# The opening of an attention block: constants built inside it, two heads prepared in separate PSUM banks, similarities ahead of scores, a weight load behind the head loop

## The reference, cut to what matters

```python
# B, H, S, D = 2, 8, 768, 64; 16 clusters
q_assign = argmax(einsum('bhsd,hcd->bhsc', q / |q|, c / |c|), axis=-1)   # k_assign likewise
mask = q_assign[:, :, :, None] == k_assign[:, :, None, :]
scores = where(mask, D ** -0.5 * q @ k.T, -1e9)
attn = softmax(scores) @ v
x = moe_1(attn, expert_emb, tau, w1, w2)      # top-1 of 8 experts
out = moe_2(x, w_gate, w1, w2)                # all 8 experts
```

## Time and profile before

| | us |
|---|---|
| median of three runs | 1681.98 |
| lowest and highest | 1680.38, 1683.75 |
| the profiled execution, its own time | 1681.38 |
| its span | 1679.4 |
| PE busy in the span | 1594.5 (95%) |
| DVE, ACT, POOL busy | 1196.2, 771.0, 277.6 |

### The profile page before, as it was taken

One profiled execution on the slowest core, in us unless ns is written; L12 is line 12 of the kernel. 1 busy time (PEld: TensorE's weight loads), 2 busy tenths in 40 slices (PEclk: granted clock), 3 DMA queues, 4 the chain that ended last, 5 costly groups with the idle time before them and its releaser, 6 DMA issues.

```text
span 1679.4 us, 27324 instructions
## 1 busy us (share of the span) xinstructions
PE 1594.5 (95%) x8554; PEld 1417.0 (84%) x8554; DVE 1196.2 (71%) x1996; ACT 771.0 (46%) x1361; POOL 277.6 (17%) x283
## 2 busy tenths in 40 slices
PE   3999999957999998999999999999999999999998
PEld 3899988846777777898998998998998998998997
DVE  3799999976899997487665665666666666666664
ACT  2576677775888885223333332322323323323331
POOL 1111111114443335010010010010010010010002
PEclk9999999988999999999999999999999999999999
DMA  3322222133353341011010010010010010010001
GB/s 71 103 58 56 56 56 57 37 86 113 138 201 123 119 150 39 13 43 33 26 51 26 25 50 26 25 50 26 25 50 26 25 50 26 25 50 25 25 0 75
DMA packets 123697, 94.90 MB, mean 57 GB/s; under 512 B 66344, under 2 KB 101160, under 8 KB 123632
## 3 DMA queue, kind: packets, MB, share of 16 engines
q1 hardware_dynamic: 121152, 86.06, 17.1%
q0 software_dynamic: 2480, 8.13, 1.6%
HBM read 87.88 MB, written 6.29 MB: 56 GB/s over the span
## 4 chain that ended last, share of the span: by engine, by line
PE 73%; DVE 2%; ACT 1%; POOL 1%; issue 1%; DMA 1%; DVEq 0%; ACTq 0%; POOLq 0%
PE moe_bank L1170 11%; PE moe_bank L1168 11%; PE moe_bank L1169 11%; PE moe_bank L1145 9%; PE moe_bank L1148 9%; PE moe_bank L1147 9%; PE moe_bank L1089 2%; PE moe_bank L1091 2%; PE moe_bank L1090 2%; PE moe_bank L1102 2%; PE moe_bank L1104 2%; PE moe_bank L1103 2%; PE moe_bank L1041 1%; ACT moe_h_rows L1315 1%; DMA moe_x_rows<-tokens,moe_token_of_item 1%
## 5 line engine op out<-in xcount | busy, mean ns | idle before, releaser
L1705 DVE SCALAR_TENSOR_TENSOR all_x<-moe_bank,all_x 128x512 f32<-128x512 f32 x336 | 251.5, 749 | 127.5 <-PE moe_bank L1170 124.7
L1145 PE MATMUL moe_bank<-moe_x_t_hi,all_w_hi 128*128 128x384 f32 x896 | 305.1, 340 | 3.0 <-DVE all_w_lo L727 2.9
L1148 PE MATMUL moe_bank<-moe_x_t_hi,all_w_lo 128*128 128x384 f32 x896 | 303.2, 338 | 0.0
L1147 PE MATMUL moe_bank<-moe_x_t_lo,all_w_hi 128*128 128x384 f32 x896 | 302.2, 337 | 0.0
L1168 PE MATMUL moe_bank<-moe_w_hi,moe_h_hi 128*128 128x512 f32 x768 | 301.1, 392 | 0.0
L1169 PE MATMUL moe_bank<-moe_w_lo,moe_h_hi 128*128 128x512 f32 x768 | 300.7, 392 | 0.0
L1170 PE MATMUL moe_bank<-moe_w_hi,moe_h_lo 128*128 128x512 f32 x672 | 265.0, 394 | 0.0
L1145 PEld LDWEIGHTS moe_bank<-moe_x_t_hi,all_w_hi 128*128 128x128 f32 x896 | 168.6, 188 | 14.0 <-issue 3.6
L1147 PEld LDWEIGHTS moe_bank<-moe_x_t_lo,all_w_hi 128*128 128x128 f32 x896 | 168.6, 188 | 11.3
L1148 PEld LDWEIGHTS moe_bank<-moe_x_t_hi,all_w_lo 128*128 128x128 f32 x896 | 168.4, 188 | 0.0
L1868 POOL TENSOR_TENSOR moe_w_sums<-moe_dense_w_raw 128x256 f32<-128x256 f32 x32 | 23.7, 740 | 853.2 <-DVE all_w_lo L727 853.2
(11 more groups left out here) (262 smaller groups left out, 3123.7 us busy)
## 6 DMA issues: line engine op xcount, KB each, us to landing
all_w_raw<-in_moe_w SPq DMA_DIRECT2D x8, 2048.0 KB, 7.6
moe_w_raw<-in_moe_w SPq DMA_DIRECT2D x8, 2048.0 KB, 9.2
moe_dense_w_raw<-in_moe_w SPq DMA_DIRECT2D x64, 256.0 KB, 3.0
moe_dense_w_raw<-in_moe_w SPq DMA_DIRECT2D x32, 512.0 KB, 3.5
attn_q_raw<-in_q SPq DMA_DIRECT2D x32, 192.0 KB, 3.4
attn_k_raw<-in_k SPq DMA_DIRECT2D x32, 192.0 KB, 3.9
attn_v_raw<-in_v SPq DMA_DIRECT2D x16, 192.0 KB, 3.8
tokens<-all_x SPq DMA_DIRECT2D x32, 96.0 KB, 2.0
```

Of the source, the lines that this page charges most:

```text
L1145: pe.matmul(out, hi[:, s, k, :], XH[chunk][:, x, k, :], start=(start and k == 0), stop=False, skip_group_check=True)
L1147: pe.matmul(out, hi[:, s, k, :], XL[chunk][:, x, k, :], start=False, stop=False, skip_group_check=True)
L1148: mm = pe.matmul(out, lo[:, s, k, :], XH[chunk][:, x, k, :], start=False, stop=(stop and k == 1), skip_group_check=True)
L1705: dve.scalar_tensor_tensor(acc, y, PROB[:, row, bass.ds(at, 1)], acc, ALU.mult, ALU.add).then_inc(y_added, 1)
```

## The change

The constants are built by POOL within the attention block, so the barrier between the two blocks is gone and each user waits for the `made` semaphore. SP issues the loads of head 0 first, with one semaphore each for q, k and v. The rows and tau go out on ACT's queue. ACT loads the table of the exponential early with a tiny activation (`TABLE`). PE runs `warm(8)` and `warm(4)`, 512-column matmuls on ones whose result nobody reads. The stages of heads 0 and 1 go to different banks of `ps_p`, `ps_t`, `ps_s` and `ps_o`, so that they don't wait for each other. The similarities of head 0 come ahead of the first scores. The first diagonal moves from POOL to DVE. SP issues the load of `W1R` behind its loop, and ACT waits for it at step 4 of the last part.

```diff
-    with nc.Block() as block:
-        @block.gpsimd
-        def _(pool):
...
-            pool.wait_ge(made, 9 + H - 1)
-    return c, scratch_at
+    return c, scratch_at, mem.sem("const_made")
+def build_constants(pool, c, made):
...
-            rows.load(sp)
-            load(0, 0)
+            for half in range(2):
+                sp.dma_start(QR[0][:, :, half, :], qd[0:1].rearrange("o p t d -> p (o t) d")).then_inc(first_q, 16)
+            for half in range(2):
+                sp.dma_start(KR[0][:, :, half, :], kd[0:1].rearrange("o p t d -> p (o t) d")).then_inc(first_k, 16)
+            sp.dma_start(VR[0][:], vd[0:1].rearrange("o p t d -> p (o t) d")).then_inc(first_v, 16)
             load(1, 1)
...
-            sp.dma_start(W1R[:, 0:DC, :], w1[0].rearrange("(c p) f -> p c f", p=P)).then_inc(w1_loaded, 16)
             with sp.Fori(2, G // 2) as i:
...
+            sp.dma_start(W1R[:, 0:DC, :], w1[0].rearrange("(c p) f -> p c f", p=P)).then_inc(w1_loaded, 16)
...
+            pe.wait_ge(made, 3)
+            warm(WARM[0])
+            pe.wait_ge(made, IDENT)
+            pe.wait_ge(first_q, 32)
+            transpose_raw(0, 0, 4).then_inc(prep_ready, 1)
+            transpose_raw(0, 4, 2, ps_t[:, 0], 4)
+            pe.wait_ge(first_k, 32)
+            transpose_raw(0, 6, 2, ps_t[:, 0], 4).then_inc(prep_ready, 1)
+            transpose_raw(0, 8, 4, ps_t[:, 1]).then_inc(prep_ready, 1)
+            pe.wait_ge(rows.step, rows.FIRST)
+            pe.transpose(ps_o[:, 0:P], unit[:].rearrange("p o d -> p (o d)"), c["ident"][:]).then_inc(cent_ready, 1)
+            warm(WARM[1])
+            pe.wait_ge(cent_split, 4)
+            pe.wait_ge(prep_lo, 3)
+            similarities(0, 0, ps_o[:, P:P + 2 * T * NC], 0)
+            similarities(0, 0, ps_o[:, P:P + 2 * T * NC], T).then_inc(prep_ready, 1)
+            pe.wait_ge(raw_loaded[1], LOADS)
+            transpose_raw(1, 0, 4, ps_s[1][:, 0]).then_inc(prep_ready, 1)
+            transpose_raw(1, 4, 4, ps_s[1][:, 1]).then_inc(prep_ready, 1)
+            transpose_raw(1, 8, 4, ps_t[:, 1]).then_inc(prep_ready, 1)
+            scores(0, 0, 0)
+            pe.wait_ge(diag_ready, 1)
+            key_ids(ps_t[:, 0], 0)
+            key_ids(ps_p[:], 3)
+            pe.wait_ge(prep_lo, 5)
+            scores(1, 1, 0)
+            pe.wait_ge(kid_ready, 2)
+            pe.wait_ge(prep_lo, 6)
+            similarities(1, 1, ps_p[:], 0)
             pe.wait_ge(rows.step, rows.DONE)
-            pe.transpose(ps_t[:, 0, 0:P], unit[:].rearrange("p o d -> p (o d)"), c["ident"][:]).then_inc(cent_ready, 1)
-            scores(0, 0, 0)
-            scores(1, 1, 0)
-            pe.wait_ge(cent_split, 4)
-            for stage in range(3, 7):
-                prep(0, 0, stage)
-            for stage in range(4):
-                prep(1, 1, stage)
-            pe.wait_ge(max_done, 1)
-            scores(2, 2, 0)
...
+            rows.load(act)
+            act.dma_start(TAU[:, 0:1], tau.rearrange("(o n) -> o n", o=1).broadcast_to([P, 1])).then_inc(tau_loaded, 16)
             rows.roots(act)
-            for stage in range(3):
-                prep(0, 0, stage)
+            act.wait_ge(made, 4)
+            act.activation(TABLE[:], c["rank16"][:, 0:1], ACT.Exp)
...
-            act.wait_ge(w1_loaded, 16)
             for s in range(2, 12):
                 step(G // 2 - 1, s)
+                if s == 4:
+                    act.wait_ge(w1_loaded, 16)
```

More of the change, by code:

```diff
@@ L146, in scale, with write @@
         dve.wait_ge(step, self.SUMS + 6)
[L147 to L150, removed]
+    def write(self, dve, j):
+        rows, outs = self.arrays[j]
+        for out in outs:
+            raw = self.raw[j][:].rearrange("r (h d) -> r h d", d=DH) if len(out.shape) == 3 else self.raw[j][:]
+            dve.tensor_scalar(out, raw, self.s[0:rows.shape[0], 2, j:j + 1], None, ALU.mult).then_inc(self.step, 1)
 def newton(dve, step, at, x, r, out, tmp):
@@ L165, in newton, with attention @@
     dve.reciprocal(out, tmp).then_inc(step, 1)
-def attention(nc, c, q, k, v, centroids, expert_emb, tau, w1, X, L, xs, W1R, W1H, w1_loaded, w1_hi, x_stored):
+def attention(nc, c, made, q, k, v, centroids, expert_emb, tau, w1, X, L, xs, W1R, W1H, w1_loaded, w1_hi, x_stored):
     with ExitStack() as stack:
@@ L309, in _, with transpose_raw, similarities, key_ids @@
         def _(pe):
-            def transpose_raw(g, j, first, n):
+            def transpose_raw(j, first, n, out=None, at=None):
+                out, at = out if out is not None else ps_p[:], first if at is None else at
                 for m in range(first, first + n):
                     src = (QR if m < T else KR)[j][:, m % T].rearrange("p o d -> p (o d)")
-                    mm = pe.transpose(ps_p[:, (m - first) * P:(m - first + 1) * P], src, c["ident"][:])
+                    mm = pe.transpose(out[:, (m - at) * P:(m - at + 1) * P], src, c["ident"][:])
+                return mm
+            def similarities(g, j, out, first):
+                cols = bass.ds((g % H) * NC, NC)
+                for m in range(first, first + T):
+                    sims = out[:, m * NC:(m + 1) * NC]
+                    if m < T:
+                        pe.matmul(sims, HI[j][:, m, :], CHL[:, cols], start=True, stop=False)
+                        mm = pe.matmul(sims, LO[j][:, m, :], CHL[:, cols], start=False, stop=True)
+                    else:
+                        pe.matmul(sims, HI[j][:, m, :], CH[:, cols], start=True, stop=False)
+                        mm = pe.matmul(sims, HI[j][:, m, :], CL[:, cols], start=False, stop=True)
+                return mm
+            def key_ids(out, first):
+                for n in range(first, first + 3):
+                    mm = pe.matmul(out[:, (n - first) * P:(n - first + 1) * P], c["onesb"][:], DIAG[:, n, :],
+                                   start=True, stop=True)
                 mm.then_inc(prep_ready, 1)
@@ L327, in prep @@
                 elif stage == 2:
                     pe.wait_ge(prep_lo, 3 * g + 2)
[L329 to L336, removed]
-                            pe.matmul(out, HI[j][:, m, :], CHL[:, cols], start=True, stop=False)
-                            mm = pe.matmul(out, LO[j][:, m, :], CHL[:, cols], start=False, stop=True)
-                        else:
-                            pe.matmul(out, HI[j][:, m, :], CH[:, cols], start=True, stop=False)
-                            mm = pe.matmul(out, HI[j][:, m, :], CL[:, cols], start=False, stop=True)
-                    if stage == 4:
-                        mm.then_inc(prep_ready, 1)
+                    transpose_raw(j, 8, 4).then_inc(prep_ready, 1)
+                elif stage == 3:
+                    pe.wait_ge(prep_lo, 3 * g + 3)
+                    similarities(g, j, ps_p[:], 0)
+                elif stage == 4:
+                    similarities(g, j, ps_p[:], T).then_inc(prep_ready, 1)
@@ L344, in prep @@
                 elif stage == 5:
                     pe.wait_ge(diag_ready, g + 1)
[L346 to L348 removed]
+                    key_ids(ps_p[:], 0)
                 else:
                     pe.wait_ge(kid_ready, 2 * g + 1)
[L351 to L352 removed]
@@ L438, in _ @@
             mm.then_inc(experts_t, 1)
+            pe.wait_ge(max_done, 1)
+            scores(2, 2, 0)
             for s in range(14):
@@ L531, in low, with prep @@
                 return dve.tensor_tensor(out, src, hi.bitcast(F32), ALU.subtract)
-            def prep(g, j, stage):
-                tiles = ps_p[:].rearrange("p (m s) -> p m s", s=P)
+            def prep(g, j, stage, out=None):
+                tiles = (ps_p[:, 0:4 * P] if out is None or stage == 4 else out).rearrange("p (m s) -> p m s", s=P)
                 if stage < 3:
```

134 lines of the change are left out of this document (72 added, 62 removed).

## The result

The changed kernel takes 1657.09 us (median of four runs, 1654.68 to 1658.37) against 1681.88 us before, measured beside it (1680.38 to 1683.75): ratio 0.985, with a 95% interval of 0.9833 to 0.9867. That is 24.8 us less, and 0.4 us from the forecast.

A forecast was written before the change was run, and what follows sets the result against it. A chain of waits through the engines, not one engine, bounds the opening. Gains of 23.6 us to tile 2 and 0.9 to tile 3 make 24.5; 1681.4 less that is 1656.9, plus 0.6 gives 1657.5 us, range 1653 to 1664.

The forecast's parts named there:

- Barrier, loads and banks, similarities at 10.5 us: Opening, head 0: without barrier and stage waits, with earlier loads, similarities start at 10.5 us against 23.15, 12.6 us gained.
- Similarities 3.6 us, with the fall of the clock within them: Head 0's similarities: the clock falls within them, they take 3.6 us, and DVE has them at 14.1 us.
- The rise by 7 us: Opening on PE: warm matmuls with the transposes behind them should lift the clock by 7 us.
- DVE as the chain, 9.75 us: Ids to maxima of tile 2: DVE's instructions set the pace, 9.75 us, ending at 23.9 us against 47.47.
- Tile 2 to tile 3, 5.7 us at the lower level: Between maxima of tiles 2 and 3: 5.7 us at a low clock against 6.6 before, 0.9 us more gained.
- Table load and W1 at nothing: ACT's early exponential-table load and the W1 load moved behind SP's loop: neither was given any gain or price.
- Routed layers, 1 us either way: Expert layers: the shifted start may meet the clock's rise at another moment, priced at 1 us either way.
- (a): Rival: clock stays high throughout, gain 27.0 us, time 1655.0 us; chance 0.22.
- (b): Rival: clock stays low or soon falls back, PE becomes the chain, gain 20 to 21 us, 1661.5 us; chance 0.17.
- (c): Rival: rows on ACT's queue land late, up to 2.5 us on the whole chain, 1660 us; chance 0.10.
- (d): Rival: gain is given back in the head loop through a lost PE and DVE balance, up to 1675 us; chance 0.03.
- (e): Rival: slower, because W1 lands so late that ACT waits at step 4; chance 0.01.

The follow-up runs named there:

- e3: Changed kernel with the constants built in a block of their own ahead, so the barrier is back: 1660.83 us, median of four runs.
- e7: Changed kernel with the loads of centroids and experts on SP's queue ahead of q: 1657.56 us, one run.
- e2: Changed kernel with the waits between preparation stages put back for heads 0 and 1, banks still separate: 1668.88 us, one run.
- e10: The changed kernel itself, unedited, timed and profiled once more: 1658.15 us, median of five runs.
- e4: Changed kernel with the W1 load put back ahead of SP's loop: 1658.23 us, one run.
- e1: Changed kernel without the twelve warm matmuls on ones: 1659.32 us, median of four runs.
- e5: Changed kernel with the first diagonal back on POOL instead of DVE: 1656.28 us, one run.
- e8: Changed kernel with the scaling of the expert embeddings moved ahead of the ids, into DVE's idle time: 1653.80 us, one run.
- e6: Changed kernel without ACT's tiny exponential that loads the table early: 1655.58 us, one run.

## Why the prediction was right, step by step

Both profiled executions of the changed kernel are close to the forecast in time (1656.79 and 1658.57 us), and the medians, 1657.09 and 1658.15, lie on either side of 1657.5. A hit within 0.4 us is luck all the same: the same kernel spreads over 4.3 us in nine runs, and terms below missed by more than that 0.4.

**Barrier, loads and banks, similarities at 10.5 us: right** (10.32). SP at 0.78 (0.9), q at 5.34 (5.4), k at 6.98 (7.0), centroids split to 10.26 (10.4). One link was later than said: the root came at 5.23 us and not 4.6, behind the experts' landing at 3.77, and the slack of ACT took it. e3 and e7 show the barrier and the rows' place at their price at the similarities; PE's start on q alone and the similarities ahead of the scores, which the sum has in this term too, were undone in no run. e2 shows the banks as the largest part found, 11.8 us in its one run.

**Similarities 3.6 us, with the fall of the clock within them: wrong in this execution** (2.96 us, with no fall in them; the 2.7 us that I gave the higher level were 0.3 short), right in kind in others: 4.5 us in e10 and e4, where the fall came sooner than I had put it. The rise by 7 us did come (between 6.2 and 7.0 us after, before 5.3 us in e10), and without the warm matmuls (e1) it came only near 20 us. But it is not sure: in e5 and e8, with the same warm matmuls, the k transposes at 7.2 us still ran at the lower level (six in 1.54 us).

**DVE as the chain, 9.75 us: right**, 9.21 measured. Of this ids 1.56 (1.5), diagonal 0.88 (0.9), low parts 2.09 (2.25), experts 0.80 (0.9), masks and maxima 1.48 and 1.49 (1.6 each), the rest 0.91 (1.0). Each term was a little long, because durations were laid end to end where the next instruction starts some 0.08 us before the end of the last. The clock was back by 17.5 us, as assumed (18). So far the chain had gained 25.0 us at tile 2 where the sum had 23.6.

**Tile 2 to tile 3, 5.7 us at the lower level: half right.** It took 4.92 us: the clock was low from 20.5 to 24.0 us and high for the rest. The end value lies between my two levels, 5.7 and 4.1.

**Table load and W1 at nothing: right** (e6; e4 with e10).

**Routed layers, 1 us either way: mis-sized.** The landmark gain was 26.7 us where I had 24.5, and 2.5 us of the gain went in the expert layers, at two places where the clock comes back later than before. So the total of 24.4 us is right partly by two errors that cancel. In e10 the landmark gain was 25.3 us and 22.6 us were left at the end of the span. From the routed layer's first load to the end of the span it is 1318.7 us before and 1321.2 after; over the experiments it lies between 1317.9 and 1321.4, mostly near the one or near the other, with the same code. The term should have been 2.5 us either way, and about as much again between tile 3 and the routed layer (306.2 to 309.2 us).

**The rivals.** (a) did not happen: no profiled execution stayed high throughout. (b) did not either: in both profiled executions of the changed kernel the clock came back by about 18 us. Its price was also too high. e1 has the ids at 16.01 us (15.7 in the rival) and PE low until near 20 us, but DVE stayed the chain: tile 2 at 25.22 and not 27.5, tile 3 at 30.33 and not 33. Only with the waits of e2 were these passed (32.83 and 36.96). The section on HAM oscillation in TensorE: Matmul & The Clock Gate of the Trainium skill says that bursts with waits between them pay for the low level again and again; these traces agree in that the level falls again and again, at 13.7 and 20.5 us in one execution and at 11.2, 21.5 and 31.7 us in another. That waits are what brings each fall, no run here shows: PE was busy from 10.3 us on when it fell at 13.7. (c): the rows did not land late for the centroids (DVE on them at 2.51 us), only 0.6 us for the experts. (d) and (e): the windows of the loop and W1's 32 us spare speak against both.

## What to carry to other kernels

When a chain through a one-bank handover opens a kernel, price more than the waits that separate banks remove: here the four waits put back cost 11.8 us in the time (one run), with PE at the lower level behind them. Choose a landmark behind which order and engines are unchanged, and follow the gain from there to the end: here 2.5 of 26.9 us went where nothing was edited, and in another execution of the same kernel 0.6 of 23.2 us. For steps under about 2 us compare landmarks of the same stretch, in more than one execution of the unchanged kernel, before a time or one trace is believed.

## What the runs showed of the hardware

The moment at which the clock falls differs between executions of the same code: at 11.2 us in e10, within the similarities, and at 13.7 us after them in the first profile, with 1.4 us between them at tile 3 and 3.7 us at the routed layer. The granted-clock column reads 1.00 in the opening while matmuls last as they do at the 1.2 GHz level (0.21 us apart in e1, 0.11 at 2.4 GHz), until the first change that the trace holds: durations are to be believed, not the column. Matmuls with 16 columns ran at the higher level for all of their 2.6 us in one execution and fell from it after 1.0 us in another, and in e1 and before the level did not rise in the 5 us that they lasted. The product for the key ids, 128x768 in bf16, takes 0.96 us on DVE (at 14.84 us in the changed kernel) and 1.47 us on POOL (at 27.03 us).
